# Attention with a mixture of experts and a max feed-forward on one core: the second feed-forward's rows in the experts' order, gated stores without gaps, indirect stores of the output

## What is computed

```python
for t in range(S):      # attention, state per batch and head
    state = alpha[:, :, t, :, None] * state + einsum('bhd,bhe->bhde', k[:, :, t], v[:, :, t])
    y[:, :, t] = einsum('bhd,bhde->bhe', q[:, :, t], state)
x = rows of y           # 3072 tokens x 384
expert_idx = argmax(cosine(x, expert_emb) / tau); gate_w = its softmax value
for e in range(8):      # every token has one expert
    out[mask] = gate_w[mask, None] * (relu(x[mask] @ w1[e]) @ w2[e])
h = maximum(maximum(out @ m1, out @ m2), out @ m3)   # 384 to 768
result = h @ mo                                      # 3072 x 384
```

## Time and profile before

| | us |
|---|---|
| three runs, median (range) | 848.24 (847.78 to 849.92) |
| profiled execution: first to last instruction (span) | 845.8 |
| TensorE busy with matmuls | 784.4 (93% of the span) |
| VectorE, ScalarE, GpSimd busy | 409.7, 255.1, 268.3 |

### The profile page before, as it was taken

How to read it: one execution, slowest core, us unless ns; L and a number is a source line. 1 busy time by engine, 2 the same in 40 slices (tenths; PEclk the granted TensorE clock), 3 DMA queues, 4 the chain that set the end, 5 groups by cost and what they waited for, 6 DMA issues and landing times.

```text
span 845.8 us, 15211 instructions
## 1 busy us (share of the span) xinstructions
PE 784.4 (93%) x4644; PEld 670.4 (79%) x4645; DVE 409.7 (48%) x735; ACT 255.1 (30%) x555; POOL 268.3 (32%) x170
## 2 busy tenths in 40 slices
PE   2988898989938999999999999999999999999998
PEld 2766676767726999999999987688888888888887
DVE  6788888888567334343333423433333333333322
ACT  5344636346232222222222222332222212122110
POOL 3245434352013745671826757410000001000000
PEclk9799999999878999999999999999999999999999
DMA  9966887845065814533325010210101101000001
GB/s 143 250 94 86 139 105 128 102 62 106 1 230 179 331 48 178 180 118 121 133 100 195 28 40 29 85 29 19 37 19 39 38 19 47 10 27 9 9 20 47
DMA packets 128881, 75.74 MB, mean 90 GB/s; under 512 B 102648, under 2 KB 122112, under 8 KB 128832
## 3 DMA queue, kind: packets, MB, share of 16 engines
q1 hardware_dynamic: 119632, 54.88, 30.0%
q0 software_dynamic: 3328, 10.23, 3.8%
q10 hardware_dynamic: 5872, 10.03, 3.2%
HBM read 59.00 MB, written 16.12 MB: 89 GB/s over the span
## 4 chain that ended last, share of the span: by engine, by line
PE 83%; DVE 11%; issue 2%; SPq 2%; DMA 1%; ACT 0%; POOL 0%; DVEq 0%; ACTq 0%
PE bank L1334 62%; DVE UA L834 4%; PE bank L1226 3%; DVE A L789 3%; PE bank L1136 3%; PE bank L1370 3%; PE bank L1196 2%; PE bank L1216 2%; PE bank L1166 2%; PE bank L1219 2%; SPq L300 2%; PE bank L1183 1%; PE bank L1320 1%; DVE UA L827 1%; PE bank L1406 1%
## 5 line engine op out<-in xcount | busy, mean ns | idle before, releaser
L465 POOL TENSOR_TENSOR wsp<-raw,wsp 128x1536 f32 x28 | 103.8, 3729 | 93.1 <-DVE wsp L1028 93.1
L1334 PE MATMUL bank<-yh,mh 128*128 128x512 f32 x324 | 128.3, 396 | 0.6 <-ACT yh L720 0.6
L1334 PE MATMUL bank<-yh,ml 128*128 128x512 f32 x324 | 126.5, 390 | 0.0
L1334 PE MATMUL bank<-yl,mh 128*128 128x512 f32 x324 | 91.3, 390 | 0.0
L1334 PE MATMUL bank<-wsp,xh 128*128 (+1 forms) x324 | 85.3, 399 | 3.7 <-issue 3.1
L1334 PE MATMUL bank<-wsp,hTh 128*128 x432 | 81.5, 340 | 1.1 <-ACT hTh L677 1.1
L506 POOL DMA_INDIRECT yg<-expert_rows,pos_i x24 | 24.7, 1029 | 171.8 <-ACT ygs L714 164.9
L1334 PEld LDWEIGHTS bank<-wsp,hTh 128*128 128x128 f32 x432 | 73.6, 188 | 1.3 <-issue 1.3
L1334 PEld LDWEIGHTS bank<-wsp,xh 128*128 128x128 f32 x324 | 58.9, 188 | 16.2 <-issue 4.0
L1098 DVE TENSOR_TENSOR t<-bank,tm 128x512 f32<-128x512 f32 x36 | 24.9, 692 | 96.5 <-PE bank L1334 96.5
L1334 PEld LDWEIGHTS bank<-yl,mh 128*128 128x128 f32 x324 | 60.9, 188 | 12.9
(11 more groups left out here) (197 smaller groups left out, 1394.8 us busy)
## 6 DMA issues: line engine op xcount, KB each, us to landing
raw<-in_moe_w SPq DMA_DIRECT2D x16, 1536.0 KB, 8.1
expert_rows<-ye ACTq DMA_DIRECT2D x27, 192.0 KB, 2.2
nat<-in_alpha SPq DMA_DIRECT2D x32, 144.0 KB, 3.1
nat<-in_k SPq DMA_DIRECT2D x32, 144.0 KB, 3.8
nat<-in_q SPq DMA_DIRECT2D x32, 144.0 KB, 4.3
vt<-in_v SPq DMA_DIRECT2D x32, 144.0 KB, 4.6
attention_rows<-xc SPq DMA_DIRECT2D x4, 1152.0 KB, 6.0
out<-oo SPq DMA_DIRECT2D x24, 192.0 KB, 1.9
```

Of the source, the lines that this page charges most:

```text
L465: g.tensor_tensor(wsp[:, ds(to, 1), 1, n, part], raw[:, n:n + 1, part], wsp[:, ds(to, 1), 0, n, part].bitcast(f32), ALU.subtract).then_inc ...
L1334: last = mm(o, x, y, start=(n == 0), stop=(n == len(todo) - 1))
```

## The change

- **Order of rows.** The second feed-forward no longer restores the order of the tokens. It takes the rows as the experts left them, sorted by expert, and the finished rows go to their tokens by indirect stores from GpSimd (`scatter`).
- **Stores closed up.** A tile goes to a row computed on VectorE (`row_t`), so that an expert's first rows follow directly on the last expert's last used row, over the unused rows of its last tile. So a store waits for the landing of the one before it. `expert_rows` gets 385 columns: the last is the token's number. The seven fills of unused tiles go.
- **Gating at the store.** ScalarE stores `gate` once to DRAM; GpSimd gathers, for each tile, the gates of its rows (`gather_gate`), 4 bytes per partition, and `y_copy` multiplies by them. `gated` goes.
- **Direct loads.** SyncE loads the tiles of the second feed-forward, the first four once the last expert's weights are split and twelve tiles landed as stored; their tiles `yg` now lie where the staging tile was.
- **The first four lifts** move before the last down product (`end`), into the banks 0, 1, 6 and 7; the keep-warm matmuls of the border go. ScalarE makes their `yh` there too; VectorE makes their `yl` before its split of the weights and not after it.
- **Tokens.** GpSimd copies a loaded tile's token numbers out of `yg` (`keep_token`); SyncE's load of the tile four later waits for that.

```diff
@@ SyncE @@
-        for t in range(GT, MT):
-            sp.dma_start(yd[P * t:P * t + P, :], causal[:].rearrange("p c n -> p (c n)")).then_inc(y_fill, 16)
+        for n in range(2):
+            sp.wait_ge(w_lo[n], CR + 2 * (E - 1))
+        for par in range(2):
+            sp.wait_ge(y_out[par], CR + 16 * ((BT + E) // 2))
+        for t in range(BT):
+            load_y(t, t)
         for par in range(2):
             sp.wait_ge(y_out[par], stored[par])
-        sp.sem_inc(y_all, 1)
-        with sp.Fori(0, NT // 2) as g:
-            for par in range(2):
-                sp.wait_ge(f_oc, CR + 2 * g + par + 1)
-                sp.dma_start(ov[ds(2 * g + par, 1)].rearrange("o p n -> p (o n)"), oo[par][:]).then_inc(o_out[par], 16)
+        for i in range(BT, NT):
+            sp.wait_ge(f_T, CR + i - BT + 1)
+            sp.wait_ge(t_tok, i - BT + 1)
+            load_y(i, i % BT)
@@ GpSimd @@
+        def gather_gate(i):
+            if i >= 2:
+                pool.wait_ge(a_y, CR + i - 1)
+            g.indirect_dma_start(out=gs[:, i:i + 1], out_offset=None, in_=gd,
+                                 in_offset=bass.IndirectOffsetOnAxis(ap=ginv_i[:, i:i + 1], axis=0)
+                                 ).then_inc(gs_in[i % 2], 16)
...
             split_low(i, 0)
+            if i == 0:
+                pool.wait_ge(gate_out, 16)
+                gather_gate(0)
+            elif i < GT:
+                gather_gate(i)
+            else:
+                with if_flag(pool, live_t, i):
+                    gather_gate(i)
             if i:
                 split_low(i - 1, 1)
...
-        pool.wait_ge(y_all, 1)
+        def keep_token(i):
+            pool.wait_ge(yg_in[i % BT], 16 * (i // BT + 1))
+            g.tensor_copy(tok_t[:, i:i + 1], yg[i % BT][:, DM:DM + 1]).then_inc(t_tok, 1)
+        def scatter(i):
+            if i >= 2:
+                pool.wait_ge(o_out[i % 2], 16 * (i // 2))
+            pool.sem_inc(oo_free, 1)
+            pool.wait_ge(t_tok, i + 1)
+            pool.wait_ge(f_oc, CR + i + 1)
+            g.indirect_dma_start(out=out, out_offset=bass.IndirectOffsetOnAxis(ap=tok_t[:, i:i + 1], axis=0),
+                                 in_=oo[i % 2][:], in_offset=None).then_inc(o_out[i % 2], 16)
+        for i in range(BT):
+            keep_token(i)
         for i in range(NT):
-            if i >= 4:
-                pool.wait_ge(f_gs, CR + i - 3)
-            g.indirect_dma_start(out=yg[i % 4][:], ...)
+            if i + BT < NT:
+                keep_token(i + BT)
+            scatter(i)
@@ ScalarE @@
-            a.copy(ye[par][:], bank[5][:, 0:DM]).then_inc(a_y, 1)
+            a.copy(ye[par][:, DM:DM + 1], inv_i[:, ds(i, 1)])
+            act.wait_ge(gs_in[par], 8 * (i - par) + 16)
+            a.activation(ye[par][:, 0:DM], bank[5][:, 0:DM], ACT.Copy, scale=gs[:, ds(i, 1)]).then_inc(a_y, 1)
...
+            act.wait_ge(y_out[1 - par], CR + 8 * (i + par))
+            row = act.value_load(row_t[0:1, ds(i, 1)], min_val=0, max_val=NTOK)
+            act.dma_start(yd[ds(row, P), :], ye[par][:]).then_inc(y_out[par], 16)
...
+        act.dma_start(gd.rearrange("(p t) o -> p (t o)", p=P), gate[:]).then_inc(gate_out, 16)
...
+        def end(i, n):
+            for t in range(BT):
+                y_hi(0, 0, t, bank[LIFT0[t]])
+            y_copy(i - 1, 1 - n % 2)
+            y_store(i - 1, 1 - n % 2)
@@ VectorE @@
+        d.scalar_tensor_tensor(ginv_i[:], inv_f[:], float(NT), bank[5][:, MT + 1:2 * (MT + 1)], ALU.mult, ALU.add)
...
+        link(d.tensor_tensor(rw["step"][:, 0:NE], rw["off"][:, 1:E], rw["off"][:, 0:NE], ALU.subtract))
+        link(d.tensor_tensor(tcmps[:, :, 0:NE], tcmp[:, :, 0:NE], ..., ALU.mult))
+        link(d.tensor_reduce(tsum[:, 3, :], tcmps[:, :, 0:NE], AX.X, ALU.add))
+        d.scalar_tensor_tensor(row_t[:], iot[:, 0:MT + 1], float(P), tsum[:, 3, :], ALU.mult, ALU.subtract)
...
         for t in range(BT):
-            y_lo(0, 0, t, bank[4 + t])
+            y_lo(0, 0, t, bank[LIFT0[t]])
+        for w in range(3):
...
@@ TensorE @@
+        def end(i, n):
+            for half in range(2):
+                pe.wait_ge((a_relu, d_relu)[half], i)
+            for t in range(BT):
+                lift_y(0, t, bank[LIFT0[t]])
+            down(i - 1)
...
             pe.wait_ge(f_yh, BT * (bk + 1))
+            if first:
+                pe.wait_ge(f_yl, CR + BT)
...
-        keep_warm(WARM_Y)
-        for t in range(BT):
-            if t:
-                keep_warm(1)
-            lift_y(0, t, bank[4 + t])
```

More of the change, by code:

```diff
@@ L162, in build @@
     hTl = sb("hTl", [P, KF, P], f32r)
-    ye = [sb(f"ye{i}", [P, DM]) for i in range(2)]
+    ye = [sb(f"ye{i}", [P, DY]) for i in range(2)]
     ff_low = cur[0]
@@ L178, in build @@
     cur[0] = region
[L179 to L182, removed]
+    gh = [sb(f"gh{i}", [P, KF2, BT * P], f32r) for i in range(2)]
+    gl = [sb("gl0", [P, KF2, BT * P], f32r)]
+    yh = [None, sb("yh1", [P, KD, BT * P], f32r)]
+    yl = [None, sb("yl1", [P, KD, BT * P], f32r)]
+    assert cur[0] <= raw_low
+    cur[0] = raw_low
+    yg = [sb(f"yg{i}", [P, DY]) for i in range(4)]
+    yh[0] = sb("yh0", [P, KD, BT * P], f32r)
+    yl[0] = sb("yl0", [P, KD, BT * P], f32r)
+    assert cur[0] <= raw_end
+    cur[0] = raw_end
+    gl.append(sb("gl1", [P, KF2, BT * P], f32r))
     tm = [sb(f"tm{i}", [P, BT * P]) for i in range(2)]
@@ L700, in _ @@
             tile(2 * g + 1, 1)
-        act.wait_ge(y_fill, 16 * (MT - GT))
-        def end(i, n):
-            y_copy(i - 1, 1 - n % 2)
-            y_store(i - 1, 1 - n % 2)
-        with act.Fori(GT // NX, (MT + 1) // NX) as g:
-            late_tiles(act, NX * g, NX, lambda i, n: tile(i, n % 2), end)
-        def gated(bk, t):
-            act.wait_ge(yg_in[t], 16 * (bk + 1))
-            act.wait_ge(f_T, CR + BT * bk + t - 1)
-            a.activation(ygs[t % 2][:], yg[t][:], ACT.Copy, scale=gate[:, ds(BT * bk + t, 1)]).then_inc(f_gs, 1)
         def y_hi(bk, par, t, src=bank[6]):
@@ L721, in y_hi @@
                    src[:, 0:DM].rearrange("p (k n) -> p k n", k=KD)).then_inc(f_yh, 1)
+        def end(i, n):
[3 more added lines that the diff above has]
+            y_store(i - 1, 1 - n % 2)
+        with act.Fori(GT // NX, (MT + 1) // NX) as g:
+            late_tiles(act, NX * g, NX, lambda i, n: tile(i, n % 2), end)
         def ff_block(bk, par, last=False):
@@ L725, in ff_block @@
                 n = KF2 * bk + f
-                if 1 <= f <= BT and not last:
-                    gated(bk + 1, f - 1)
                 act.wait_ge(f_p, CR + 3 * n + 1)
@@ L1382, in tile, with lift_y @@
             turn_h(i)
+        def lift_y(bk, t, dst=None):
+            pe.wait_ge(yg_in[t], 16 * (bk + 1))
+            if dst is None:
+                dst = bank[6]
+                pe.wait_ge(f_yl, CR + BT * bk + t)
+            for kk in range(KD):
+                last = tr(dst[:, P * kk:P * kk + P], yg[t][:, P * kk:P * kk + P], ident[:])
+            last.then_inc(f_T, 1)
+        def end(i, n):
[4 more added lines that the diff above has]
+            down(i - 1)
         pe.wait_ge(w0_lo, NU - UPB)
@@ L1395, in _ @@
         with pe.Fori(GT // NX, (MT + 1) // NX) as g:
-            late_tiles(pe, NX * g, NX, lambda i, n: tile(i, n, g), lambda i, n: down(i - 1))
-        def lift_y(bk, t, dst=None):
-            pe.wait_ge(f_gs, CR + BT * bk + t + 1)
-            if dst is None:
-                dst = bank[6]
-                pe.wait_ge(f_yl, CR + BT * bk + t)
-            for kk in range(KD):
-                last = tr(dst[:, P * kk:P * kk + P], ygs[t % 2][:, P * kk:P * kk + P], ident[:])
-            last.then_inc(f_T, 1)
+            late_tiles(pe, NX * g, NX, lambda i, n: tile(i, n, g), end)
         def out_product(bk, par, t, dst):
@@ L1424, in ff_block @@
                 for w in range(3):
+                    if first and f == 1 and w == 2:
+                        pe.wait_ge(f_m1, CR + 1)
                     if first and f in (0, KF2 // 2):
```

67 lines of the change are left out of this document (35 added, 32 removed).

## The result

The changed kernel takes **873.88 us** (median of four runs, 871.12 to 875.27), the kernel before beside it 848.55 (four runs): a ratio of 1.0284, 95% interval 1.0259 to 1.0309. I had forecast 852.2, in a range of 841.5 to 859. The profiled execution has a span of 872.6 for 845.8, 26.8 us more.

A forecast was written before the change was run, and what follows sets the result against it. TensorE, with 83% of the last chain, was taken to bound the kernel, the 13.4 us border being what could be won. Terms -10.2 + 6.8 + 1.3 + 3.5 + 1.4 + 1.2 = +4.0 gave 852.2 us, range 841.5 to 859.

The forecast's parts named there:

- The border: Between the last down product and the second feed-forward's first product: TensorE starts the latter 10.2 us sooner, at 527.85.
- GpSimd's queue: At the border: flag tests and splits delay the tokens, so TensorE stalls 6.8 us for tile 4's load (0.7 to 7.9).
- The hold-up between VectorE and GpSimd: During the splits of the second weights: VectorE's three casts add 3 x 0.97 = 2.9 us to GpSimd's splits.
- The clock: After TensorE's idles before and in the second feed-forward's first block: lower clock costs +1.3 us (between 0 and 2.8).
- Gates of tile 0: At the first expert tile: its gates land late behind weights in flight, TensorE waits +3.5 us (0 to 4.3).
- Gates where experts open: At five tiles opening an expert: late gates cost 2.7 us together, halved to +1.4 (0 to 5.1).
- The last store: At the kernel's end: an indirect store lands later than the direct store's 1.9 us, +1.2 us (0 to 2.2).
- At nothing: Router's table work, row-number loads, removed fills and gating, added GpSimd issues, loads waiting for scatters: all put at no cost.
- A: Tokens hardly late: tests at 0.3, splits not held up, no cold clock; -3.4, 844.8 us; chance 0.22.
- B: Small gathers land soon (3.0 us) whatever is in flight, both gate terms vanish; -0.9, 847.3 us; chance 0.15.
- C: Everything late, nearly all costs at their upper ends; +12.1, 860.3 us; chance 0.10.

The follow-up runs named there:

- e12: The changed kernel with one wait more, so VectorE splits the second weights only after GpSimd has finished its own splits: 873.69 us.
- e4: The kernel before plus one indirect load by GpSimd after the last output copy, its data unused, SyncE waiting for it: 856.21 us.
- e2: The changed kernel with 32 unused bytes ahead of the large tiles, so the weight slots lie at a multiple of 64: 871.02 us, ratio 1.0258.
- e5: The changed kernel with the first four keep_token ahead of GpSimd's splits of the second weights: 866.86 us.
- e3: The changed kernel with the gather of gates ahead of split_low(i, 0) in GpSimd's order for tiles 0 to 23: 863.57 us.
- e6: The changed kernel with gates gathered two tiles ahead over four semaphores, before the split: 850.31 us.
- e7: The changed kernel with gates two tiles ahead, keep_token before the splits and 32 bytes of padding together: 850.97 us against 849.09 for the kernel before, ratio 1.0017.
- e8: As e7, with 64 bytes of padding behind ye so that ml and ol lie at multiples of 128: 851.62 us, ratio 1.0026.
- e1: The kernel before with 480 unused bytes per partition ahead of the large tiles: 849.58 us against 848.79, ratio 1.0008.
- e9: The kernel before with the second feed-forward's tiles in the places the change gives them, computing as before: 850.28 us.

## Why the prediction was wrong

The direction held and so did the mechanism that I named for it, the queue of GpSimd; the size was 22 us short. Two steps failed most: the cost of that queue, and the last store, which left out GpSimd's DRAIN. By the steps:

- **The border**, -10.2: measured -10.9 from the last down product on and +0.4 at the last tiles, -10.5. Right, with its wait for yl.
- **GpSimd's queue**, +6.8: measured +12.0. This step failed, in two terms. Tests at 0.5 us each: they cost 0.7, above the 0.57 that I had held for the upper end. From the issue of the last gather to the splits are 11.5 us and not 8.0. That is 3.5 of the 5.2 missed; a start of the queue 0.5 later in relation to the border, and splits of 27.9 and not 27.0, are most of the rest. The 0.57 was 10.8 us divided by 19 tests, and the 19 was miscounted from the code: the trace of before has the loads of GpSimd's sequencer by line, and I didn't open that view. Between 487.3 and 498 they are 2 + 10 + 1 (instruction, count, ns min/median/max, first and last start):

```profile
L262 POOLq TENSOR_LOAD <-live_t x2: 286/494/703, 489.0 to 491.6; - x2
```
```profile
L459 POOLq TENSOR_LOAD <-first_t x10: 284/287/293, 487.6 to 496.1; - x10
```
```profile
L495 POOLq TENSOR_LOAD <-free_t x1: 288/288/288, 496.8 to 496.8; - x1
```

  So "no row shows one alone" was untrue: thirteen in 9.8 us, from 487.6 to 497.4, make 0.75 each, and the forecast's own sum with it would have been 3.8 us higher, 856.0.
- **The hold-up between VectorE and GpSimd**, inside that term: I priced it by one DMA issue beside a cast and on GpSimd alone. The trace shows both engines held: where both ran without a break, a pair of passes on each took 6.06 us, with 0.96, 1.36, 2.11 and 2.65 for the four when apart (e12). The Trainium skill (SBUF — State Buffer, SBUF: two separate sides) says that GpSimd and a VectorE instruction that uses their shared pair of ports take it as an exclusive lock for the whole instruction. The trace agrees in kind: VectorE's cast starts at 544.84 and ends 0.8 behind GpSimd's pass that ends at 546.88. By strict turns the four would be 7.08, the trace has 6.06.
- **The clock**, +1.3: measured +2.7, the upper bound (2.8). A second low stretch, after the wait of 3.72, lies hidden in the stall.
- **Gates of tile 0**, +3.5: +3.3. Right. The landing took 6.1, and 5.6 in the median of all 27. The Trainium skill (DMA: Bandwidth & Descriptors, Anatomy of one DMA) has about 2.0 us for such a DMA; only the quickest landing, 2.4, is near that.
- **Gates where experts open**, +1.4: +3.6, inside its range. "These few bytes may slip through" was wrong: of the 2.2 missed, 1.3 come from halving 2.7.
- **The last store**, +1.2: +6.0, far outside. This step failed too. For what it counted, until SyncE has seen the stores, it was right: +1.3. But the program ends with its own instructions, and GpSimd's DRAIN adds 4.7, which stood nowhere in the sum. It was in the trace of before at 717.5, with 5507 ns, and I didn't read it because it was hidden. I had moved GpSimd's last DMA to the end without asking what GpSimd does behind it.
- **At nothing**: the blocks (+3.6) and the ordinary tiles (+0.6). That the tiles' places could matter to a matmul I hadn't considered. The rest that I had put at nothing stayed there: the router took 0.3 more, loads waited for no scatter.
- **Not a step at all**: +5.5 before the first down product, in this trace; e4 has 5.2 of it without the change. But the medians lie 25.3 apart, 4.0 more than the 21.3 of the terms, so the untraced runs of the changed kernel carry something of this size as well. Whether it's attention's clock or the low clock at tile 1, which e2, e5 and e12 show, is open.

Added up on the trace: the forecast's +4.0 becomes +21.3 by the terms above, and 5.5 by what comes before. Rivals A and B fell: the tests cost what they cost, and small gathers don't land soon beside weights. C, everything late, had the right sign and was still 14 us short. In the trace it's 14.7: 4.1 in GpSimd's queue, 3.8 at the end, 4.6 in blocks and tiles and 5.5 before the first down product, less 3.3 that it had too high elsewhere.

Left open: 1.7 us of the blocks; 4 us between the medians and the terms; and why a place in the memory changes a matmul's pace at all.

## What to carry to other kernels

When an instruction that waits is put into an in-order queue, read all that is queued behind it until the next engine is due, and give it a place where its own wait is long over: moving gathers two tiles ahead was worth some 20 us here. Price what is skipped as well (0.7 us a flag test on GpSimd), and let no split of one of VectorE and GpSimd be planned beside the other's at its lone length. Before the last DMA moves to another engine, read that engine's instructions at the program's end.

## What was not expected of the hardware

- GpSimd's DRAIN at the program's end takes 7.7 us where its last work was an indirect store (nine traces, 7716 to 7719 ns), 5.5 to 5.6 after an indirect load, 4.8 after a cast; VectorE's takes 0.6. It starts before the engine's last DMA is shown as issued.
- A wait of 3.05 us was followed by a full clock (changed kernel, 285 to 305), waits of 3.13 (e2, e12) and 3.08 (e5) at the same instruction by 1.2 GHz, 2.6 to 2.8 us lost. After the 2.5 at the border e3, e6, e7 and e8 fell too; the changed kernel, e2, e5 and e12 did not.
- A matmul's pace hangs on where its operands lie: the weight slots at byte 32352 for 31872 cost 0.035 of 9.5 us (e1), and at 32384 nothing (e2); the second feed-forward's tiles moved cost 0.27 of 24.7 in one block (e9).
